# Attention, mixture of experts and feed-forward on one core: a load held back behind two landings, a weight piece held behind the row numbers, four scatters under way, and a combine placed ahead of two weight splits

## What is computed

```
attn:  k_p, v_p = mean of 8 neighbouring rows of k and v       # 8 x 8 heads, 576 rows, 64 wide
       x = softmax(q k_p^T / 8) v_p                            # 4608 tokens x 512
moe:   noisy = x w_gate + log(1 + exp(x w_noise)) * noise      # 8 experts
       the two largest of noisy, softmax over the two
       out = sum over both of weight * relu(x w1[e]) w2[e]     # 512 -> 1024 -> 512
ffn:   h = x w_in;  out = (h - tanh(h)) w_out                  # 512 -> 2048 -> 512
```

## Time and profile before

| | us |
|---|---|
| median of 3 runs | 1939.85 |
| lowest and highest of them | 1936.11, 1949.44 |
| the profiled execution | 1927.76 |
| its span in the trace | 1926.1 |
| PE busy in it | 1889.9 (98%) |
| DVE busy | 996.3 (52%) |
| POOL busy | 519.3 (27%) |
| median landing of the 32 loads of 1 MB of expert weights | 5.0 |

### The profile page before, as it was taken

The page is one execution under the profiler, slowest core; times in us unless marked ns, Lnnn a source line. Parts: engine busy times, 40 slices in busy tenths (PEclk is TensorE's granted clock), DMA queues, the critical chain, the costliest instruction groups (busy, mean ns, idle before and its releaser), DMA issues.

```text
span 1926.1 us, 35567 instructions
## 1 busy us (share of the span) xinstructions
PE 1889.9 (98%) x13106; PEld 1722.4 (89%) x13107; DVE 996.3 (52%) x1920; ACT 818.8 (43%) x1719; POOL 519.3 (27%) x507
## 2 busy tenths in 40 slices
PE   8999899999999999999999999999999999999999
PEld 7989888998999999999989888999999999999998
DVE  5888733314132131312213186666777777776665
ACT  6988523324132232323223254444444444444444
POOL 2245442222112121111121332222322222222222
PEclk9999899999999999999999999999999999999999
DMA  9988324414122131311313121011100000000000
GB/s 213 222 199 179 106 81 142 142 45 142 44 87 92 49 136 49 130 44 65 109 61 135 66 77 34 33 34 55 41 33 33 33 33 33 33 33 33 33 33 22
DMA packets 94360, 152.22 MB, mean 79 GB/s; under 512 B 18912, under 2 KB 62048, under 8 KB 91488
## 3 DMA queue, kind: packets, MB, share of 16 engines
q1 hardware_dynamic: 70304, 100.24, 17.1%
q0 software_dynamic: 24000, 51.26, 9.7%
HBM read 110.54 MB, written 40.40 MB: 78 GB/s over the span
## 4 chain that ended last, share of the span: by engine, by line
PE 84%; DMA 6%; POOL 3%; issue 3%; DVE 3%; SPq 1%; ACT 0%; POOLq 0%; ACTq 0%; DVEq 0%
PE banks L867 14%; PE banks L866 13%; PE banks L865 13%; PE banks L856 13%; PE banks L857 13%; PE banks L858 13%; DMA slot_row<-row_w,slot_w 4%; PE banks L846 3%; POOL slot_row L543 2%; DMA k_raw<-in_k 1%; DVE w_lo L1424 0%; PE banks L749 0%; POOL v_raw L514 0%; PE banks L892 0%; PE banks L894 0%
## 5 line engine op out<-in xcount | busy, mean ns | idle before, releaser
L856 PE MATMUL banks<-x_hi,w_hi 128*128 128x256 f32 x2304 | 637.3, 277 | 3.1 <-DVE g L1573 2.1
L857 PE MATMUL banks<-x_lo,w_hi 128*128 128x256 f32 x2304 | 636.8, 276 | 0.0
L858 PE MATMUL banks<-x_hi,w_lo 128*128 128x256 f32 x2304 | 636.7, 276 | 0.0
L865 PE MATMUL banks<-w_hi,h_hi 128*128 128x512 f32 x1184 | 468.6, 396 | 3.0 <-DVE h_lo L1526 3.0
L867 PE MATMUL banks<-w_hi,h_lo 128*128 128x512 f32 x1184 | 466.9, 394 | 0.0
L866 PE MATMUL banks<-w_lo,h_hi 128*128 128x512 f32 x1184 | 464.4, 392 | 0.0
L856 PEld LDWEIGHTS banks<-x_hi,w_hi 128*128 128x128 f32 x2304 | 432.8, 188 | 6.0 <-DVE g L1573 2.7
L857 PEld LDWEIGHTS banks<-x_lo,w_hi 128*128 128x128 f32 x2304 | 432.8, 188 | 2.5
L858 PEld LDWEIGHTS banks<-x_hi,w_lo 128*128 128x128 f32 x2304 | 433.0, 188 | 0.0
L689 POOL TENSOR_SCALAR large<-u_sq 128x512 uint8<-128x512 f32 x144 | 222.5, 1545 | 571.1 <-ACT u_sq L1176 304.3
L1450 DVE SCALAR_TENSOR_TENSOR h_lo<-banks,h_hi 128x512 fp32r<-128x512 f32 x144 | 99.6, 692 | 360.3 <-ACT h_hi L1106 351.6
(11 more groups left out here) (169 smaller groups left out, 2051.5 us busy)
## 6 DMA issues: line engine op xcount, KB each, us to landing
w_raw<-in_moe_w SPq DMA_DIRECT2D x32, 1024.0 KB, 5.0
y<-y_rows SPq DMA_DIRECT2D x17, 1024.0 KB, 5.1
q_sb<-in_q SPq DMA_DIRECT2D x32, 288.0 KB, 6.2
x_rows<-x_sb SPq DMA_DIRECT2D x32, 288.0 KB, 5.1
out_x<-y_sb SPq DMA_DIRECT2D x36, 256.0 KB, 2.1
k_raw<-in_k SPq DMA_DIRECT2D x16, 288.0 KB, 5.7
v_raw<-in_v SPq DMA_DIRECT2D x16, 288.0 KB, 7.5
w_raw<-in_moe_w_in SPq DMA_DIRECT2D x4, 1024.0 KB, 4.8
```

The source lines that it names most:

```text
L856: pe.matmul(part, hi, x_hi[:, c, :], start=(c == 0), stop=False)
L857: pe.matmul(part, hi, x_lo[:, c, :], start=False, stop=False)
L858: mm = pe.matmul(part, lo, x_hi[:, c, :], start=False, stop=(c == NC - 1))
L865: pe.matmul(p_y[m][:, :], hi, w_hi[par][:, o:o + DM], start=(j == 0), stop=False)
```

## The change

1. SP, batch 0: in front of `load_k(1, 1)` it waits until the first parts of k and v of batch 1 have landed. Everything that stands behind it in SP's queue (`load_v(1, 1)`, `load_q(1, 1)` and on) waits with it.
2. POOL: the four transfers that prepare the tables are issued one batch later.
3. SP, batch 7: in front of weight piece 2 it waits until `rows_a` has landed.
4. The scatters signal over four semaphores, not two. In the loop over the batches there are still two under way; from the one behind the first early gather on there are four (`under_way`).
5. First block of the feed-forward: DVE combines the next block ahead of the last two splits, not behind them, and PE transposes the result in front of down tile 14, not 13.

```
-        scattered = [sem(f"scattered{i}") for i in range(2)]
+        scattered = [sem(f"scattered{i}") for i in range(LANDINGS)]      # LANDINGS = 4
...
                     load_q(b + 1, 0)
+                    if is_first(b):
+                        sp.wait_ge(k_in[0], 48)
+                        sp.wait_ge(v_in[0], 48)
                     load_k(b + 1, 1)
                 if not is_first(b):
                     store_x(b - 1, 2)
                 if is_last(b):
+                    sp.wait_ge(rows_a_in, 16)
                     sp.wait_ge(split_lo, 4)
                     load_w(2, w_src(0, 2))
...
-            def scatter(b, begin, end):
+            def scatter(b, begin, end, under_way=2):
...
                     k = b * WAY + n
-                    wait(pool, scattered[k % 2], 16 * (k // 2))
+                    if k >= under_way:
+                        done = k - under_way
+                        pool.wait_ge(scattered[done % LANDINGS], 16 * (done // LANDINGS + 1))
                     pool.indirect_dma_start(slot_row, bass.IndirectOffsetOnAxis(ap=slot_w[b % 2][:, n:n + 1], axis=0),
-                                            row_w[:, b, n:n + 1], None).then_inc(scattered[k % 2], 16)
+                                            row_w[:, b, n:n + 1], None).then_inc(scattered[k % LANDINGS], 16)
...
-                if b == 0:
+                if b == 1:
                     pool.dma_start(slot_row.rearrange("(p n) o -> p (n o)", n=COLS), dump_i[:, :, :].rearrange("p b m -> p (b m)")).then_inc(zeroed, 16)
...
-            scatter(B - 4, SOME, WAY)
+            scatter(B - 4, SOME, WAY, LANDINGS)
...
-                scatter(b, 0, WAY)
+                scatter(b, 0, WAY, LANDINGS)
...
-                    if j == FT2 - 3 and not last_c:
+                    if j == (FT2 - 2 if is_first(cb) else FT2 - 3) and not last_c:
                         turn(comb, cb + 1, ct_done)
...
                 if is_first(cb):
-                    for i in range(SPLIT_FIRST + FP2 - SPLIT_FROM, FT2):
+                    for i in range(SPLIT_FIRST + FP2 - SPLIT_FROM, FT2 - 2):
                         split(E + 1, i, 1)
                 if not last_c:
                     combine(cb + 1)
+                if is_first(cb):
+                    for i in range(FT2 - 2, FT2):
+                        split(E + 1, i, 1)
+                if not last_c:
                     turned(cxhi, cb, cxlo)
```

More of the change, by code:

```diff
@@ L61, in attention_moe_ffn @@
     FROM = B - 4
+    LANDINGS = 4
     AHEAD = 2
@@ L307, in landed @@
         def landed(b, i):
-            return 16 * (((b + 1) * WAY + 1 - i) // 2)
+            return 16 * (((b + 1) * WAY + LANDINGS - 1 - i) // LANDINGS)
         block = ctx.enter_context(nc.Block())
@@ L377, in load_slots @@
                 if b >= 2:
-                    for i in range(2):
+                    for i in range(LANDINGS):
                         sp.wait_ge(scattered[i], landed(b - 2, i))
```

## The result

| | before | changed |
|---|---|---|
| median of 10 runs each, one chip, us | 1935.63 | 1943.93 |
| lowest and highest | 1930.73, 1949.44 | 1941.76, 1948.12 |
| profiled execution (its span) | 1927.76 (1926.1) | 1948.12 (1946.4) |

The ratio is 1.004, 95% interval [1.0021, 1.0058]: 8 us slower, where 16.4 us less were forecast; the range ended at 1938.

The account below looks back on a forecast made before the run. PE, busy 1889.9 of 1926.1 us, was taken to set the end, with four waits of 13.4 us to save. Terms 4.6 + 2.6 + 5.8 + 3.4 = 16.4 us, from the median 1939.85, gave 1923.4; range 1914 to 1932, over all cases 1910 to 1938.

Parts of the forecast that it names:

- term 3: Tail scatters: four under way bring the third expert block's rows earlier, removing PE's 4.14 us wait; 5.8 us, ends 1.5, 5.8.
- Term 1: Attention batch 0: holding loads back lands POOL's add earlier, shortening PE's 3.94 us wait; 4.6 us, ends 0 and 6.0.
- Term 2: Batch 7: weight piece 2 behind the row numbers shortens DVE's 4.60 us wait; 2.6 us net, ends 0 and 4.6.
- Term 4: First feed-forward block: combining before the last splits shortens PE's 2.29 us wait; 3.4 us, ends 1.0 and 3.7.
- A: Rival: transfers share instead of queueing, so terms 1 and 2 give nothing and piece 2 is late; 1932.7, chance 0.20.
- C: Rival: POOL's scatters get behind, delaying row numbers and weight piece 2; slower, 1946.5 at 1.0 us a pair; chance 0.05.
- D: Rival: waits shift to the next late thing each time, nothing left beyond 2 us; 1938, chance 0.08.
- The signs that I named for being wrong: Adds over 8 us again, DVE waiting for k's second part at batch 1's start, or scatters, four at a time, over 6.

Follow-up runs that it names:

- P: Chip of follow-up runs on scatters in the tail; the kernel before took 1930.49 us there.
- S: Chip of follow-up runs; the kernel before took 1917.28 us there, the changed kernel 1910.74, ratio 0.9964.
- two in the tail: Changed kernel with two scatters under way in the tail, as before, not four: 1930.13, ratio 1.0013 on P; 1914.57, ratio 0.9985 on S.
- Load alone: Kernel before with edits 1 and 2 alone, on R: 1918.61 us, ratio 1.0008 [0.9994, 1.0022].
- piece alone: Kernel before with edit 3 alone, weight piece 2 behind the landing of the row numbers, on Q: 1930.52 us, ratio 0.9985.
- four alone: Kernel before with edit 4 alone, four scatters under way in the tail, on P: 1945.64 us, ratio 1.008.
- combine alone: Kernel before with edit 5 alone, on R: 1914.95 us, ratio 0.9979 [0.9965, 0.9993].
- T: Chip of follow-up runs; the kernel before took 1919.01 us there, the changed kernel 1909.98, ratio 0.9948.
- the bursts: Changed kernel, tail scatters in bursts of four, each behind the landing of the last: 1926.06, ratio 0.9963 on Q; 1927.32, ratio 1.0043 on S.
- Q: Chip of follow-up runs on pace, bursts and edit 3; the kernel before took 1933.32 us there.
- R: Chip of follow-up runs on single terms and pauses; the kernel before took 1918.67 us there.

## Why the prediction was wrong

**The step that failed is in term 3**: that scatters issued closer together cost the other engines nothing. The trace of before did hold seven back to back (256.7 to 264.3) with PE busy, so the row spoke for it; on the chip of the verdict it was not so. Edit 4 alone costs 15 us on P (1945.64 against 1930.49, ACT standing 34.5 us in all). On S it gains 1914.57 - 1910.74 = 3.8 us. Even there its working was off. I let a landing take 4.7 us, but that median is of two transfers only, the two reads of the table (7.05 and 2.39 us); no scatter is in it. By the semaphores a scatter of that trace takes 2.1 to 2.2 us in quiet stretches, where at 1.27 apart two are under way whatever is allowed, and up to 5.6 beside loads in the tail. What the permission removes is the gaps of that second kind. The last scatter came at 252.0, earlier than the 257.7 I worked out, and then PE's own work set the start at 266.6. The 5.8 counted the wait of 4.1, which goes (3.94 in two in the tail on S, now 0), and 1.7 of clock, which isn't seen. But in this pair of profiles the third block starts only 0.64 us earlier (266.64 against 267.28), since PE gets there later; the 3.8 us is the runs' figure.

**Term 1 gave 0, not 4.6.** Load alone is 1.0008 [0.9994, 1.0022], 1 us faster to 4 slower. The wait of 3.94 was that execution's: piece alone, four alone and the kernel below, without edits 1 and 2 too, have 1.49, 1.97 and 0.59 there. The kernel with only the combine moved, whose attention is that of before, shows PE and the chain like this:

```profile
29.50 1.22 PE L749 MATMUL banks<-vp,pT 128*96 128x81 f32 x12 [0.59 <-DVE x_sb L1278]
```
```profile
11.20 8.94 DMA k_raw<-in_k
...
20.87 6.21 DMA k_raw<-in_k
```

The load took 8.94 and the add 6.21 us, not 10.22 and 8.54, with the same loads queued between. The eleventh division of the attention (DVE `x_sb`) starts at 53.1 in the profile of before, at 47.2 to 49.6 in the five others without edits 1 and 2, and at 47.1 to 51.3 with them. There was little to gain. In the changed kernel's chain the add is short, 5.85 us, but issued later, and lands at 27.7, where it lands at 27.1 above (start, us, what):

```profile
13.29 8.54 DMA v_raw<-in_v
21.89 5.85 DMA k_raw<-in_k
```

**Term 2's mechanism was right.** DVE and SP in order of time in the changed kernel, answering to the earlier trace rows; then the landing of the row numbers:

```profile
197.82 0.17 DVE L1425 TENSOR_SCALAR large<-large 128x4 int32<-128x4 int32 x1 [0.16 <-DVE slot_i L1380]
...
199.94 0.63 SPq L336 DMA_DIRECT2D w_raw<-in_moe_w  x1
```
```profile
large<-slot_row POOLq DMA_DIRECT2D x1, 2.0 KB, 1.9
```

1.9 us and not 7.1, so DVE's 4.60 is gone, more than the 3.6 I took. It holds on the other kind too: combine alone, without edit 3, has a landing of 6.1 and DVE waiting 4.25 us, and the kernels with edit 3 on S and T have landings of 1.9 to 3.1 and waits of 0.16 to 0.29. Piece 2 then is late by this, on chip S (I had 1.0):

```profile
204.31 0.63 ACT L1091 ACTIVATE w_hi<-w_raw 128x512 fp32r<-128x512 f32 x1 [1.87 <-DMA w_raw<-in_moe_w]
```

By itself it measured 0.9985 [0.9965, 1.0005], 3 us, with no gain at all inside the interval; with edit 5 on S both give 0.9991, less than edit 5 alone on R. What I left out is that PE waits at the third block anyway, for the last scatter: 4.0 to 4.5 us in the quiet kind's kernels with neither edit 3 nor 4, so an earlier end of batch 7 counts only as far as POOL too is earlier (last scatter 256.2 with it and 257.8 without, on different chips).

**Term 4 held.** PE's wait went from 2.29 to 0.53 (0.3 was forecast), with the clock at 1.00 around it (1150 to 1165); combine alone gave 0.9979 [0.9965, 0.9993], which is 4.0 us, for 3.4. And the stretch from the third block to the end is 1645.3 us on average over the 15 profiles with the edit, 1648.5 over the 5 without: 3.2 less.

**The sum** of 16.4 becomes 0 + (0 to 3) + 3.8 + 3.3, 7 to 10, where no engine stands still; measured 0.9964 and 0.9948, that is 7 and 10 (6.5 and 9.0 by the medians). Taking the sum from 1939.85 mixed the trace of one kind of chip with the runs of the other: the 12.1 us between them, which I took for spread of the runs, are by the record counts at least in part the difference between the kinds.

**Rivals.** A is out for term 2: without the megabyte the 2 KB land in 1.9 to 3.1. The round-robin rule of the Trainium skill (DMA: Bandwidth & Descriptors, Queues, rings and completion order) would allow this too, since it is silent on how long a read takes once the megabyte is gone; these runs don't decide between it and order of issue. C has the right sign and the wrong mechanism: POOL got ahead, not behind, and PE paid. D came out for term 1 and in part for term 2. The signs that I named for being wrong would not have told. DVE doesn't wait for the second part of k, and scatters landing in over 6 us do show at the start of the tail (7.8 and 6.7 us in the changed kernel's first timing), but on S just the same (8.3, 7.4 and 6.3), where it was the fastest. I had named no sign on PE during the tail itself.

**What stays open** is what holds PE up. Shown: it goes with a nearly unbroken run of scatters, on some chips; the number allowed matters only through the run (piece alone stands still with two, the bursts hardly with four); PE's rows and signals are late while DVE and ACT do what waits for nobody at their usual length; the transfers are nearly idle (share 0.02 from 220 to 230). Not shown: whether PE lacks instructions, as its single matmuls "issue" suggest. The page counts as many packets of instructions on each queue in the changed kernel as before (32 and 24), which speaks neither for it nor against. Nor is it shown that it would happen without the recording.

## What to carry to other kernels

Before you price a wait, look at it in more than one execution: one of four here was not the kernel's. Before you read a landing from semaphore records, count them, and ask of a median how many and which transfers it is of. A change worth under 1% that lets one engine issue faster wants its timing on more than one chip; here the same kernel is 0.4% slower on one and 0.4 to 0.5% faster on two others. When all engines stand still together with idle transfers, look at what the one busy engine issues, and break its run to test it.

## What the runs showed of the hardware

- Indirect scatters of 128 numbers issued every 1.27 us by POOL went with PE's standstills of 2 to 11 us at a time in the first timing and on P and Q (34.5 us of ACT's waits in one tail of 34 scatters), and with none over 2 us on R, S and T.
- Breaking the run did away with nearly all of it: 1.88 us apart, 4.2 us left; bursts of four with a landing between, 5.7 left. One memset of 89 ns between (1.34 apart) left 23.3.
- A scatter of 128 numbers lands in 2.1 to 2.2 us when little else moves, and beside loads in up to 5.6 at 209 us of the kernel before and 8.3 at 202.5 of the changed kernel on S. With plain writes of the same size between them, POOL waited 44.8 us for 34 of those.
- The chips fell in two groups: kernel before 1930 to 1936 us and 974 to 1686 DMA semaphore records missing of some 8000, against 1917 to 1919 us and 20 to 52 missing. Whether the lost records, the recording or something else of the chip goes with the standstills as a cause isn't shown.
